# Routing in a fused attention and mixture-of-experts kernel: POOL conversions moved out of the chain, token counts summed on TensorE, marks in 16 bits

## The reference

```python
# attention: 2 batches, 8 heads, 768 tokens, head dim 64; a 6-bit hash masks the scores
q_bits, k_bits = (q @ proj > 0), (k @ proj > 0)        # 6 bits each, packed to a bucket
scores = where(q_bucket == k_bucket, q @ k.T / 8, -1e9)
x = softmax(scores) @ v                                # to rows of 512
# 8 experts, the best one for each token
logits = x @ w_gate                                    # 1536 x 8
expert_idx = argmax(logits, axis=1)
gate_w = probs[arange(N), expert_idx]                  # softmax of the logits
for e in range(8):
    xe = x[expert_idx == e]
    out[expert_idx == e] = gate_w * (maximum(xe @ w1[e], 0) @ w2[e])   # 512 -> 1024 -> 512
# dense layer 512 -> 2048 -> 512 with ELU
h = out @ w_in
y = where(h > 0, h, exp(minimum(h, 0)) - 1) @ w_out
```

## Time and profile before

| | |
|---|---|
| median of 3 runs | 829.99 us (827.31 to 830.59) |
| the profiled execution | 828.12 us, of which the trace spans 826.3 |
| PE busy | 780.2 us (94%) |
| DVE busy | 422.7 us (51%) |
| ACT busy | 341.7 us (41%) |
| POOL busy | 366.8 us (44%) |
| mean granted TensorE clock | 0.981 |

### The profile page before, as it was taken

The page is one execution under the profiler, slowest core; times in us unless marked ns, Lnnn a source line. Parts: engine busy times, 40 slices in busy tenths (PEclk is TensorE's granted clock), DMA queues, the critical chain, the costliest instruction groups (busy, mean ns, idle before and its releaser), DMA issues.

```text
span 826.3 us, 13915 instructions
## 1 busy us (share of the span) xinstructions
PE 780.2 (94%) x4106; PEld 661.7 (80%) x4107; DVE 422.7 (51%) x746; ACT 341.7 (41%) x686; POOL 366.8 (44%) x463
## 2 busy tenths in 40 slices
PE   5899999999999449999999999999999999999996
PEld 4799999999999338888888888888888888888885
DVE  5888888898888664212212222233334443343332
ACT  5778777877788313122222222222222222222221
POOL 3334433543444443999999999139000100010001
PEclk9999999999999859999999999999999999999998
DMA  6566574364463436676666765412000100010001
GB/s 158 129 188 177 135 208 114 94 159 115 110 199 108 156 128 214 201 206 197 188 200 205 238 205 178 158 51 90 14 14 14 51 1 1 1 51 1 1 0 52
DMA packets 73302, 97.24 MB, mean 118 GB/s; under 512 B 33264, under 2 KB 36080, under 8 KB 73264
## 3 DMA queue, kind: packets, MB, share of 16 engines
q1 hardware_dynamic: 63344, 76.56, 33.1%
q10 hardware_dynamic: 7760, 13.07, 4.9%
q0 software_dynamic: 2160, 7.09, 2.3%
HBM read 59.57 MB, written 19.44 MB: 96 GB/s over the span
## 4 chain that ended last, share of the span: by engine, by line
PE 83%; DVE 5%; issue 4%; DMA 3%; ACT 2%; SPq 1%; POOL 1%; DVEq 1%; POOLq 0%; ACTq 0%
PE ps_s L694 14%; PE ps_s L696 14%; PE ps_s L695 14%; PE ps_t L787 5%; PE ps_t L786 5%; PE ps_t L785 5%; PE ps_t L636 5%; PE ps_s L621 3%; PE ps_s L622 2%; PE ps_p L601 2%; PE ps_o L653 2%; PE ps_o L652 2%; PE ps_t L723 2%; DVE stats L1053 1%; PE ps_p L586 1%
## 5 line engine op out<-in xcount | busy, mean ns | idle before, releaser
L576 POOL DMA_INDIRECT out_dram<-out_sb,token_of x12 | 11.8, 980 | 234.5 <-ACT out_sb L945 231.8
L875 ACT ACTIVATE probs<-ps_s,stats 128x768 f32<-128x768 f32 x96 | 95.5, 995 | 41.7 <-POOL stats L474 40.9
L1066 DVE TENSOR_TENSOR pt_lo<-ps_t,pt_hi 128x384 fp32r<-128x384 f32 x192 | 96.9, 546 | 7.1 <-ACT pt_hi L866 6.9
L1053 DVE TENSOR_REDUCE stats<-ps_s 128x1 f32<-128x768 f32 x96 | 91.5, 953 | 16.1 <-PE ps_s L622 15.4
L866 ACT ACTIVATE pt_hi<-ps_t 128x384 fp32r<-128x384 f32 x192 | 83.7, 490 | 13.0 <-PE ps_t L636 12.5
L472 POOL TENSOR_SCALAR stats<-stats 128x1 f32<-128x1 f32 x96 | 21.2, 221 | 137.6 <-DVE stats L1053 137.5
L525 POOL TENSOR_TENSOR w_lo<-stage,w_hi 128x1024 fp32r<-128x1024 f32 x34 | 81.4, 2396 | 0.0
L636 PE MATMUL ps_t<-ident,probs 128*128 128x128 f32 x576 | 79.8, 274 | 1.3 <-DVE pt_lo L1066 1.2
L954 ACT ACTIVATE elu_e<-elu_e 128x512 f32<-128x512 f32 x48 | 30.3, 632 | 115.5 <-DVE elu_e L1277 115.5
L694 PE MATMUL ps_s<-w_hi,gT_hi 128*128 128x512 f32 x192 | 76.5, 398 | 0.0
L525 POOL TENSOR_TENSOR w_lo<-late_stage,w_hi 128x1024 fp32r<-128x1024 f32 x32 | 76.4, 2398 | 0.0
(11 more groups left out here) (184 smaller groups left out, 1685.3 us busy)
## 6 DMA issues: line engine op xcount, KB each, us to landing
stage<-in_moe_w_dram SPq DMA_DIRECT2D x72, 256.0 KB, 3.2
late_stage<-in_moe_w_dram SPq DMA_DIRECT2D x56, 256.0 KB, 3.4
key_hi_hi<-query_hi_mask SPq DMA_DIRECT2D x30, 192.0 KB, 3.8
x_slots<-x_rows SPq DMA_DIRECT2D x19, 257.0 KB, 5.0
y_dense<-y_sb ACTq DMA_DIRECT2D x19, 256.5 KB, 3.9
xg<-x_slots ACTq DMA_DIRECT2D x16, 257.0 KB, 4.3
raw_qk<-in_q_dram SPq DMA_DIRECT2D x16, 192.0 KB, 3.2
raw_v<-in_v_dram SPq DMA_DIRECT2D x16, 192.0 KB, 2.7
```

Source lines behind the costliest of these rows:

```text
L875: a(probs[:, s % 4].rearrange("p (h c) -> p h c", h=2), ps_s[:, 2 * (s % 2):2 * (s % 2) + 2, 0:HW], ACT.Exp, bias=stats[:, 2, c], scale=st ...
L1053: v_.tensor_reduce(stats[:, 0, c], ps_s[:, 2 * (s % 2):2 * (s % 2) + 2, 0:HW], AX.XY, ALU.max).then_inc(max_found, 1)
L1066: v_.tensor_tensor(pt_lo[gb][where], ps_t[:, half, 0:HW].rearrange("p (t c) -> p t c", c=P), pt_hi[gb][where].bitcast(F32), ALU.subtract). ...
```

## The change

**Choice.** The sum of the logits over the first seven heads is made ahead of the last head's; afterwards one addition is left. Comparing and multiplying are one instruction. `chosen` is laid out by token tile, with one zero tile behind the twelve. The last head's copy to `x_rows` moves from ahead of the sum to behind the choice, and its store to `x_tokens` from SP to ACT's queue.

**Counting.** One accumulation in PSUM: `before` times all of `chosen`, then twelve matmuls of `ones`, each with `chosen` shifted by one more token tile. Tile t of the result is then the place within the tile plus the counts of all earlier tiles, and the zero tile gets the totals. The copy, the eight scans, the subtraction and the addition on DVE go. DVE reads both from PSUM.

**Marks.** `slot_of` is bfloat16, and a slot tile is marked by twelve TENSOR_SCALARs, one for each token tile, with the token's slot as a scalar from memory.

**Order.** POOL converts nothing of expert 1; ACT and DVE do all eight chunks. POOL issues gather 0, four scatters, gather 1, four scatters, gather 2, four scatters. The first scatter now waits for the gate (`rt_gate`), which DVE makes behind `find(0)`. `w_ready` is raised in three steps of 4, 2 and 2. TensorE runs mark 2's matmuls behind the first half of slot tile 0.

```diff
-        slot_of, c = place("slot_of", [P, P], F32, c)
+        slot_of, c = place("slot_of", [P, P], BF16, c)
...
-        chosen, c = place("chosen", [P, E, TT], BF16, c)
+        chosen, c = place("chosen", [P, TT + 1, E], BF16, c)
...
-                    if isinstance(before, int) and before == 0 and c >= 4 + EARLY:
-                        sp.wait_ge(early_lo, c - 3 - EARLY)
+                    if isinstance(before, int) and before == 0 and c >= 4:
+                        sp.wait_ge(early_lo, c - 3)
                     elif not (isinstance(before, int) and before + c < 4):
                         sp.wait_ge(w_ready, before + c - 3 + W_START)
                     elif c == 2:
                         early_rows = slice(QT, TT)
                         sp.wait_ge(prep_moved, CHUNKS - 1)
                         sp.dma_start(x_token_rows[:, early_rows, 0:DM - D], x_rows[:, early_rows, 0:DM - D]).then_inc(x_stored, 16)
-                        sp.wait_ge(prep_moved, CHUNKS)
-                        sp.dma_start(x_token_rows[:, early_rows, DM - D:DM], x_rows[:, early_rows, DM - D:DM]).then_inc(x_stored, 16)
                         sp.wait_ge(rt, 1)
                     load_stage(sp, c % 4, *tiles_of(c))
...
-            pool.wait_ge(prep_moved, CHUNKS)
-            convert(0, EC * CH, end=EARLY)
             pool.wait_ge(slots_clear, 16 * ST)
             g.tensor_copy(x_rows[:, :, DM + 1], iota_i[:, m_i:m_i + TT]).then_inc(tokens_set, 1)
             pool.wait_ge(tokens_set, 1)
             pool.wait_ge(x_stored, 16 * 3)
-            for k in range(DIRECT):
-                pool.wait_ge(rows_made, k + 1)
-                g.indirect_dma_start(out=x_direct[:, k], out_offset=None, in_=x_tokens,
-                                     in_offset=bass.IndirectOffsetOnAxis(ap=rows_of[:, k:k + 1], axis=0)).then_inc(direct_in[k], 16)
-            pool.wait_ge(rt_pos, 1)
             for t in range(TT):
+                if t % (TT // DIRECT) == 0:
+                    k = t // (TT // DIRECT)
+                    pool.wait_ge(rows_made, k + 1)
+                    g.indirect_dma_start(out=x_direct[:, k], out_offset=None, in_=x_tokens,
+                                         in_offset=bass.IndirectOffsetOnAxis(ap=rows_of[:, k:k + 1], axis=0)).then_inc(direct_in[k], 16)
+                if t == 0:
+                    pool.wait_ge(rt_gate, 1)
                 g.indirect_dma_start(out=x_slots, out_offset=bass.IndirectOffsetOnAxis(ap=pos[:, t:t + 1], axis=0),
                                      in_=x_rows[:, t], in_offset=None).then_inc(scattered, 16)
-            pool.wait_ge(early_lo, EC - EARLY)
-            pool.sem_inc(conv_hi, EC - EARLY)
-            pool.sem_inc(w_ready, EC - EARLY)
+            pool.wait_ge(early_lo, EC // 2)
+            pool.sem_inc(w_ready, EC // 2)
+            pool.wait_ge(early_lo, EC - 2)
+            pool.sem_inc(w_ready, 2)
...
+            pool.wait_ge(early_lo, EC)
+            pool.sem_inc(conv_hi, EC)
+            pool.sem_inc(w_ready, 2)
...
-            pe.wait_ge(prep_moved, CHUNKS)
             pe.wait_ge(rt, RT_CHOSEN)
-            flat = chosen[:, :, :].rearrange("p e t -> p (e t)")
-            mm(ps_o[:, 0:TT * E], before[:], flat, start=True, stop=True).then_inc(rt_count, 1)
-            mm(ps_p[:, 0:TT * E], ones[:], flat, start=True, stop=True).then_inc(rt_count, 1)
+            flat = chosen[:, :, :].rearrange("p t e -> p (t e)")
+            mm(ps_o[:, 0:(TT + 1) * E], before[:], flat, start=True, stop=False)
+            for shift in range(1, TT + 1):
+                last = mm(ps_o[:, shift * E:(TT + 1) * E], ones[:], flat[:, 0:(TT + 1 - shift) * E], start=False, stop=shift == TT)
+            last.then_inc(rt_count, 1)
             found = [ps_t[:, 0, 0:2], ps_t[:, 1, 0:2], ps_p[:, 0:2]]
-            for k in range(DIRECT):
+            def find_rows(k):
                 for t in range(TT):
                     if t % QT == 0:
                         pe.wait_ge(slots_marked, k * 2 + t // QT + 1)
                     last = mm(found[k], is_slot[:, k, t], token_parts[:, t], start=t == 0, stop=t == TT - 1)
                 last.then_inc(rows_found, 1)
+            find_rows(0)
+            find_rows(1)
...
+                if first:
+                    find_rows(2)
...
+            act.wait_ge(prep_moved, CHUNKS)
+            act.dma_start(x_token_rows[:, QT:TT, DM - D:DM], x_rows[:, QT:TT, DM - D:DM]).then_inc(x_stored, 16)
...
-            act.wait_ge(prep_moved, CHUNKS)
-            for c in range(EARLY, EC - 2):
+            act.wait_ge(weighted, HEADS * 2)
+            for c in range(EC // 2):
                 early_high(c)
             move_xg(0, 0)
...
+                if with_early:
+                    early_high(with_early)
+                    early_high(with_early + 1)
...
+                if isinstance(i, int) and i == PAIRS:
+                    return
...
+                        if isinstance(i, int) and i == PAIRS:
+                            v_.memset(chosen[:, TT], 0.0)
+                            v_.tensor_reduce(LG[:, QT:TT], logit_parts[:, 0:H - 1, QT:TT].rearrange("p h t e -> p t e h"), AX.X, ALU.add)
                         move_rows(i, h - 1)
...
-            step(add_logits(1))
+            step(v_.tensor_tensor(LG[:, QT:TT], LG[:, QT:TT], logit_parts[:, H - 1, QT:TT], ALU.add))
...
-            step(v_.tensor_tensor(te[0], LG[:], over_e(top), ALU.is_equal))
-            step(v_.tensor_tensor(te[1], te[0], over_t(ev[:]), ALU.mult))
+            step(v_.scalar_tensor_tensor(te[1], te[2], 0.0, over_t(ev[:]), ALU.is_equal, ALU.mult))
             step(v_.tensor_reduce(best, te[1], AX.X, ALU.max))
-            step(v_.tensor_tensor(chosen[:, :, :].rearrange("p e t -> p t e"), over_e(best), over_t(ev[:]), ALU.is_equal))
+            step(v_.tensor_tensor(chosen[:, 0:TT], over_e(best), over_t(ev[:]), ALU.is_equal))
             assert done[0] == RT_CHOSEN
-            dve.wait_ge(rt_exp, 1)
-            step(v_.tensor_reduce(total, te[3], AX.X, ALU.add))
-            step(v_.tensor_tensor(small[:, 3, 0:TT], total, tiny[:], ALU.add))
-            step(v_.reciprocal(x_rows[:, :, DM], small[:, 3, 0:TT]))
-            dve.wait_ge(rt_count, 2)
-            step(v_.tensor_copy(r[4], ps_p[:, 0:TT * E]))
-            for e in range(E):
-                last = v_.tensor_tensor_scan(et[5][:, e], scan_one[:], et[4][:, e], 0.0, ALU.mult, ALU.add)
-            step(last)
-            step(v_.tensor_tensor(r[6], r[5], r[4], ALU.subtract))
-            counts = et[5][:, :, TT - 1:TT].to_broadcast([P, E, TT])
-            step(v_.tensor_tensor(et[7], counts, jv[:].rearrange("p (o t) -> p o t", o=1).to_broadcast([P, E, TT]), ALU.is_gt))
-            filled, upto, start = small[:, 4, 0:E], small[:, 5, 0:E], small[:, 6, 0:E]
+            dve.wait_ge(slots_clear, ST * 16)
+            v_.tensor_tensor(x_rows[:, QT:TT, DM - D:DM], ps_p[:, 0:QT * XR].rearrange("p (t c) -> p t c", c=XR)[:, :, 0:D],
+                             inv[:].rearrange("p (t o) -> p t o", o=1).to_broadcast([P, QT, D]), ALU.mult).then_inc(prep_moved, 1)
+            dve.wait_ge(rt_count, 1)
+            ahead, counts = ps_o[:, 0:TT * E].rearrange("p (t e) -> p t e", e=E), ps_o[:, TT * E:(TT + 1) * E]
+            step(v_.tensor_tensor(et[7], counts.rearrange("p (e o) -> p e o", o=1).to_broadcast([P, E, TT]),
+                                  jv[:].rearrange("p (o t) -> p o t", o=1).to_broadcast([P, E, TT]), ALU.is_gt))
+            filled, upto, start, padding = small[:, 4, 0:E], small[:, 5, 0:E], small[:, 6, 0:E], spare[:, 1, 0:E]
             step(v_.tensor_reduce(filled, et[7], AX.X, ALU.add))
             step(v_.tensor_tensor_scan(upto, scan_one[:, 0:E], filled, 0.0, ALU.mult, ALU.add))
             step(v_.tensor_tensor(start, upto, filled, ALU.subtract))
-            step(v_.tensor_tensor(r[6], r[6], ps_o[:, 0:TT * E], ALU.add))
-            step(v_.scalar_tensor_tensor(et[0], start.rearrange("p (e o) -> p e o", o=1).to_broadcast([P, E, TT]), float(P), et[6],
-                                         ALU.mult, ALU.add))
-            step(v_.tensor_tensor(et[1], et[0], chosen[:], ALU.mult))
-            step(v_.tensor_reduce(small[:, 7, 0:TT], et[1].rearrange("p e t -> p t e"), AX.X, ALU.add))
+            step(v_.scalar_tensor_tensor(te[0], over_t(start), float(P), ahead, ALU.mult, ALU.add))
+            step(v_.tensor_tensor(te[1], te[0], chosen[:, 0:TT], ALU.mult))
+            step(v_.tensor_reduce(small[:, 7, 0:TT], te[1], AX.X, ALU.add))
             slots = small[:, 7, 0:TT]
             def mark(k):
-                for half in range(2):
-                    ts = slice(half * QT, half * QT + QT)
-                    v_.scalar_tensor_tensor(is_slot[:, k, ts], slots[:, ts].rearrange("p (t o) -> p t o", o=1).to_broadcast([P, QT, P]), float(k * P),
-                                            slot_of[:].rearrange("p (o s) -> p o s", o=1).to_broadcast([P, QT, P]),
```

(29 more changed lines are left out.)

43 lines of the change are left out of this document (20 added, 23 removed).

## The result

The changed kernel takes **810.4 us** (median of 4 runs, 810.0 to 811.4) against 830.3 for the kernel before beside it: ratio 0.977 [0.9745, 0.9795], 19.9 us less. The forecast was 822.0 with a range from 819.0 to 826.5, so the sign was right and the gain was forecast at less than half its size. A ratio in this text is a kernel's time over that of the kernel before, run beside it, with its 95% interval in brackets.

What follows compares the result with a forecast made beforehand. After attention a routing hole of some 21 us on DVE's chain, then TensorE bounds. Net 8.1 us off the profiled 828.12 gives 820.0; the median's 1.87 us above gives 822 us, range 819 to 826.5.

Steps and rivals of the forecast that it cites:

- choice written: DVE's routing after the last logits: five steps of 0.29 us write the choice at 282.11, against 288.17 before.
- Marks of a tile: Twelve 16-bit TENSOR_SCALARs on DVE mark a slot tile in 2.1 us, against 1.83 before.
- Transposes: TensorE's transposes ahead of the first expert matmul start at 293.05 by either path, against 301.68: 8.6 us won.
- Mark 2's matmuls: Twelve TensorE matmuls moved behind the first half of slot tile 0, costing 0.5 us there.
- the store of the last 192 KB: DMA of x_rows, moved to ACT's queue: lands in 2.6 us, at 285.4, before the first gather wants it at 287.7.
- the sum of the routing: From last logits to first expert matmul: 8.6 us won, less 0.5 for mark 2, net 8.1 us.
- what must not come late: Behind the first expert matmul: gather 1, early_low, last scatter and POOL's conversions stay in time; expert 7 has 4.1 us spare.
- the last step of the sum: Whole kernel: the median of the runs lies 1.87 us above the profiled execution, taking 820.0 to 822 us.
- A: DVE's marks run at one element a cycle, 3.3 us a tile; 2.3 us of gain go, 824.3; chance 0.12.
- D: TensorE's clock stays at 1.2 GHz through tile 0's output, costing 9.6 us: 831.5, slower than before; chance 0.04.
- C: DVE's three slow routing steps are slow by themselves, two keep 2.3 us; 4.1 us less gain, 826; chance 0.04.
- B: DVE and POOL hold each other up around marks and scatters, delaying gather 1; 825.5; nil if only two-SBUF-input instructions do; chance 0.16.

Runs made afterwards that it cites:

- the kernel with the old pace: The changed kernel with 32 bytes more ahead of the routing and expert tiles and x_rows 32 bytes later: ratio 0.985 to the kernel before.
- the run with POOL busy: The changed kernel with four added POOL instructions beside the routing, two of one input and two of two, results unused: 816.6 us in one execution.
- old marks: The changed kernel with the kernel before's marks, two f32 instructions with two SBUF inputs instead of twelve 16-bit ones: 813.9 us, ratio 0.9805.

## Why the prediction was wrong

**The routing, step by step, was right.** Counted from the last logits (0.49 us later in the new trace): choice written 1.88 predicted, 1.97 measured to the end of L1150. First mark 4.74, measured 4.48: the counts took 0.5 us and not 0.8. Marks of a tile 2.1, measured 2.04 (2.29 beside the first scatter). Rows at 7.25, measured 6.94; gather issued at 8.41, measured 8.20. Transposes at 12.82, measured 12.23, behind mark 1's matmuls and not behind the gather, as said. From there 2.75 us to the first expert matmul, said 2.74. Mark 2's matmuls, priced at 0.5, cost nothing: tile 0's second half starts 6.64 us behind the first expert matmul in both kernels, twelve slow matmuls in both. They lie where TensorE waited for ACT's `hid` and its transposes took 0.95 us to the next start, now 0.57. One term was off without showing: the store of the last 192 KB took 4.7 us to land and not 2.6, and the first gather waited for it last ([13.02 <-DMA x_tokens<-x_rows]); it cost 0.1 us. So the sum of the routing, 8.1, should have been 9.2; the kernel with the old pace measured 8.99 over the whole stage.

**The step that failed** stands in the first paragraph: "Whatever starts the first expert matmul earlier moves the end by the same amount, as long as nothing behind it comes late." The list of what must not come late was right, no conversion and no load came late. But I had asked only what could be later, and took for granted that 2064 matmuls whose code is untouched keep their pace. The diff moves their operands by 32 bytes, and I read those lines as bookkeeping. The missing term, from the changed kernel's paces: 912 x 0.0039 in the experts, 384 x 0.0069 for yT and 384 x 0.0065 for gT in blocks 0 and 2, 192 x 0.0043 for gT in block 1, together 9.5 us; the trace has 8.7 there. The term was put at nothing, and it is most of the miss of 11.6 us. The rest: 1.1 from the routing, and 2.0 from the last step of the sum, which put the median 1.87 us above the profiled execution, as before, where it now lies 0.13 below it; attention, which ended 0.5 us later, takes a little of this back. From the trace of before alone its size could not be told, since all distances in it are slow ones. That it could move was to be seen: the offsets differ in the diff, and TensorE was said to be the bound.

**The rivals.** A (marks at one element a cycle) and D (the clock stays low) did not come: marks at 2.04, and the granted clock, 0.50 up to 300 us, is 1.00 from 302 us on. C is out by the run with POOL busy. B came nearly in the form in which I had called it nil: the 16-bit marks did not hold POOL up, the instructions with two SBUF inputs did, behind gather 1. Beside the 16-bit marks a scatter takes 1.01 us, beside `w_lo` 2.25:

```profile
290.44 1.01 POOL L553 DMA_INDIRECT x_slots<-x_rows,pos  x1 [0.30 <-issue]
...
298.22 2.25 POOL L553 DMA_INDIRECT x_slots<-x_rows,pos  x1 [0.30 <-issue]
```

Gather 1 was issued at 295.57, before those, so TensorE did not wait in tile 0. The Trainium skill (SBUF — State Buffer, "SBUF: two separate sides") would have the 16-bit marks as the worse neighbour, since a 2-port mode takes the ports from POOL's descriptor writing. The measurement is the other way round, 1.01 us beside the marks against 2.25 beside `w_lo`. This does not refute the rule: no run shows in which mode the marks ran, and each lasts only 0.25 us. Nor does the delay beside `w_lo`: by the Trainium skill (the same section) two SBUF inputs matter against a POOL instruction that reads SBUF, and an indirect DMA that reads its row numbers there may count as one, which no run here shows.

**What the range lacked.** It was built of mechanisms inside the routing. With the offsets' term, between 0 and some 10 us, it would have reached down to 810.

## What to carry to other kernels

When a change resizes or moves a tile, list the start of every tile that TensorE reads behind it, in the old layout and the new, and compare the pace of matmuls whose code is untouched before you credit the change with the time. Where TensorE is the bound, give the two operands of a long fp32r matmul stage the same start modulo 256 bytes, and measure it: here 128 bytes of gaps in the kernel before are worth 1.3% of the kernel. Then look at what feeds that stage, for a faster TensorE uses up the lead of the others. Cost a change by undoing its side effects one at a time: with the old paces put back, this one is worth 9 us of the stage and not 18.

## What the runs showed of the hardware

- The pace of a 512-column fp32r matmul at full clock hangs on the distance between the starts of its two SBUF operands: 0.2265 to 0.228 us in a dense block whose operands all start at the same place modulo 256 bytes, 0.233 at most other distances. Moving all tiles by 32 bytes together changes nothing. This is shown by moving tiles alone, in both directions; the mechanism behind it is not known.
- A stationary operand 64 bytes below the moving one costs 0.229 and 64 above it 0.233. Why, and why xgT at distance 0 stays at 0.2284, no run tells.
- A small DVE step with two SBUF inputs that runs beside a POOL elementwise instruction ends when that one does (0.70 to 2.32 us against 0.26); a DVE reduction with one input stays at 0.25.
- DVE instructions with two SBUF inputs hold POOL's indirect DMAs up (1.48 to 3.26 us against 0.97, the longest in the changed kernel with 32 bytes more). The DVE instructions are not longer for it: old marks 1.81 us for two beside them, 1.83 alone. Twelve TENSOR_SCALARs on 16 bits with one SBUF input did not hold POOL up (1.01 us); beside the scatters their last one took 0.50 us instead of 0.25, at an unchanged pace.
- A DVE TENSOR_SCALAR on 128 16-bit elements takes 0.10 us from one start to the next, 0.16 with a scalar read through a pointer. An estimate from the Trainium skill (VectorE: DVE Perf Modes, "The TRN2 errata"), which has no term for a pointer, is 94 ns: near the first, well under the second.
